# Phase angles by batch: the shared middle tile multiplied and transposed in two 64-row halves

## The chip, the cores and the metric

The kernel runs on one core of one Trainium2 chip. The metric is the device time of one execution in microseconds (us), lower is better. The kernel before takes 2743.87 us (median of 3 runs, 2742.2 to 2744.56). Engines are named as the profile names them: PE is TensorE (its matmuls), PEld are TensorE's weight loads, DVE is VectorE, ACT is ScalarE, POOL is GpSimd, SP is SyncE, which issues most DMAs.

## The reference, cut to what matters

```python
# x: (4, 4224, 192); weight: (8, 7)
def _attn_ref(x, weight):            # causal 7-tap convolution along the sequence, taps softmaxed, one set per head
    ...
def _moe_ref(x, w_theta, w_tok_r, w_tok_i, w_ch):
    theta = x @ w_theta              # (4, 4224, 192): the phase angles
    zr = x * np.cos(theta)
    zi = x * np.sin(theta)
    y = w_tok_r @ zr + w_tok_i @ zi  # two 4224 x 4224 token mixings, for each batch
    u = x + y
    return u + np.maximum(u @ w_ch, 0.0)
def _moe2_ref(x, U, V, w_ch1, w_ch2):
    h = x.transpose(0, 2, 1) @ U @ V # low rank (32) token mixing
    u = x + h.transpose(0, 2, 1)
    return u + np.maximum(u @ w_ch1, 0.0) @ w_ch2   # 192 -> 768 -> 192

out = _moe2_ref(_moe_ref(_attn_ref(x, weight), ...), ...)
```

The change touches only the angles `x @ w_theta` and the token-major copy of `x` that is multiplied with their sine and cosine. Everything is float32.

## The kernel before

**Layout.** The four batches are handled as two pairs. A pair has 2 x 192 = 384 channels, which lie on three tiles of 128 partitions: tile 0 holds channels 0 to 127 of the first batch, tile 1 (the shared one) channels 128 to 191 of the first batch on partitions 0 to 63 and channels 0 to 63 of the second on partitions 64 to 127, tile 2 channels 64 to 191 of the second batch. Tokens run along the free dimension. `Y` keeps the running sum for all four batches and 4224 tokens in SBUF.

**Three stages.** (1) From 0 to about 2130 us 385 steps (`STAGES`) of the token mixing: each step multiplies one operand `z_op` (tokens as the contraction) with one block of weights, as 27 float32r matmuls (lines 1276 to 1278: high x high, high x low, low x high part). Odd and even steps take PSUM banks 0 to 2 and 3 to 5. ACT writes the high part of the weights (line 586), DVE the low part (line 943), DVE adds the finished banks to `Y` (lines 969 to 983). The order of all work on all engines is written out by stage number. (2) The channel mixing `u @ w_ch` and the projection on U (lines 1292 to 1327). (3) The second channel network (lines 1356 to 1375).

**The work around the change.** The operands are prepared in 22 groups of 384 tokens of one pair (`GP`), each in three units of 128 tokens (`KC`), 66 units in all, spread over the steps of stage 1 up to 1886 us. DVE computes the convolution into `attn` (lines 868 and 871); for unit m PE runs `theta(n, r)`, all in plain float32, which PE executes as two records for each matmul, each with a weight load of its own, and as one record for each transpose:

- line 1220: tile 1 (all 128 rows) with `theta_w[:, D:3D]` into all 384 columns of the angle bank; this part of the matrix has the first batch's weights on rows 0 to 63 and columns 0 to 191, the second's on rows 64 to 127 and columns 192 to 383, and zeros elsewhere
- line 1221: tile 0 into columns 0 to 191; line 1224: tile 2 into columns 192 to 383
- line 1226: three transposes of `attn` tiles into the x bank; the last one releases ACT.

Then ACT rounds the angles to turns (`turn`, lines 605 and 608), DVE reduces them (`angles`, lines 907 to 911), ACT computes sines (`sin`, lines 615 to 620) and DVE multiplies them with the x bank (`products`, lines 920 and 922). The results go to DRAM and come back as the operands of later steps. Units 0, 1 and 2 run before the first step, their banks are listed in `theta_bank` and `x_bank`; all later units use bank 6 for the angles and bank 7 for x. A unit waits for the products of the unit before (`pe.wait_ge(product, 2 * m)`). The two float32 convolution tiles that PE computes at the start are line 1234, in `conv_pe`.

One other place has a 64-row matmul: `spread_g` (line 1312), run twice in the whole kernel, multiplies `spread` (64 partitions, 96 columns) with `g_parts` in plain float32. `low_rank` (line 1308) contracts over 96 partitions.

Of the kernel before, what the change touches and what calls it, by code (L numbers as in the profile page):

```python
# [8 lines left out]
ACT = mybir.ActivationFunctionType  # L9
ALU = mybir.AluOpType  # L10
AX = mybir.AxisListType

P = 128
BATCH, SEQ, D = 4, 4224, 192
TAPS, HEADS, RANK, FF = 7, 8, 32, 768
PAIRS = BATCH // 2
TP = 2 * D // P
TILES = PAIRS * TP
TOK_TILES = SEQ // P
GW = 384  # L20
# [10 lines left out]
INV_2PI = float(np.float32(1 / (2 * np.pi)))  # L31
ROUND = 12582912.0
TWO_PI_A = 6.28125
# [70 lines left out]
def splits_done(o):  # L104
    return KC * (o + 1) if o < PIECED else KC * PIECED + o - PIECED + 1
# [54 lines left out]
def conv_done(n):  # L160
    return 2 * TAPS * (n + 1) if n < 2 else 4 * TAPS + CONV * (n - 1)
# [60 lines left out]
def zf_index(m):  # L222
    return m if m < KC else (m % 2 if m < FIRST_UNITS else 0)


def zf_stores(m):
    same = [i for i in range(min(m, FIRST_UNITS - 1) + 1) if zf_index(i) == zf_index(m)]
    return len(same) + max(m - FIRST_UNITS + 1, 0)


def unit_before(m):
    return m - KC + 1 if m == KC - 1 else m - 1
# [31 lines left out]
def build(nc, w_tok, xin, taps_w, w_theta, w_ch, u, v3, w1, w2, ident_in, spread_in, z_out, out):  # L264
    top = ExitStack()
    with top:
        def sb(stack, name, shape, dt=F32):
            return stack.enter_context(nc.sbuf_tensor(name, shape, dt))

        def sem(name):  # L270
            return top.enter_context(nc.semaphore(name))

        psum = top.enter_context(nc.psum_tensor("bank", [P, 8, 512], F32))
# [3 lines left out]
        ident = sb(top, "ident", [P, P])  # L277
# [4 lines left out]
        theta_w = sb(prep, "theta_w", [P, 4 * D])  # L282
# [3 lines left out]
        angle = sb(prep, "angle", [P, GW])  # L286
# [82 lines left out]
        angle_step = sem("angle_step")  # L369
        sin_step = sem("sin_step")  # L370
        product = sem("product")
# [54 lines left out]
        def zf_of(m):  # L426
            return (zf, zf_1, z_raw[:, 1])[zf_index(m)]

        def turns_of(m):
            return turns_1 if m == 1 else turns  # L430

        def angle_of(m):
            return sines_1[:, 0] if m == 1 else angle

        def sines_of(m):
            return sines_1 if m == 1 else sines

        def theta_bank(m):
            return psum[:, {1: 3, 2: 5}.get(m, 6), 0:GW]

        def x_bank(m):
            return psum[:, {1: 4, 2: 2}.get(m, 7), 0:GW]


        @block.sync
# [130 lines left out]
        def _(act):  # L576
# [24 lines left out]
            def turn(m):  # L601
                act.wait_ge(theta_ready, m + 1)
                if m >= 2:
                    act.wait_ge(angle_step, 3 * unit_before(m) + 3)
                nc.scalar.activation(turns_of(m)[:], theta_bank(m), ACT.Copy, scale=INV_2PI,
                                     bias=ROUND).then_inc(turn_step, 1)
                act.wait_ge(turn_step, 2 * m + 1)
                nc.scalar.activation(turns_of(m)[:], turns_of(m)[:], ACT.Copy, bias=-ROUND).then_inc(turn_step, 1)
# [49 lines left out]
            for n, t in enumerate((2, 0)):  # L658
                for k in range(TAPS):
                    nc.scalar.activation(diag[n][:, k], ident[:], ACT.Copy,  # L660
                                         scale=tap[:, t, k:k + 1]).then_inc(diag_ready, 1)
            nc.scalar.activation(sines[:, 0, 0:1], tap[:, 0, 0:1], ACT.Sin).then_inc(table_ready, 1)
            w_hi(0)
            copy_conv(0)
            turn(0)
            turn(1)
            sin(0)
            turn(2)
            piece_hi(0, 0)
            copy_conv(1)  # L670
# [163 lines left out]
        def _(dve):  # L834
            vec = nc.vector
# [64 lines left out]
                        vec.tensor_tensor(h, h, there, ALU.add).then_inc(residual, 1)  # L900

            def angles(m):
                theta, a, t = theta_bank(m), angle_of(m), turns_of(m)
                dve.wait_ge(turn_step, 2 * m + 2)
                if m >= 2:
                    dve.wait_ge(sin_step, 4 * unit_before(m) + 2)
                vec.scalar_tensor_tensor(a[:], t[:], -TWO_PI_A, theta, ALU.mult, ALU.add).then_inc(angle_step, 1)
                dve.wait_ge(angle_step, 3 * m + 1)
                vec.scalar_tensor_tensor(a[:], t[:], -TWO_PI_B, a[:], ALU.mult, ALU.add).then_inc(angle_step, 1)
                dve.wait_ge(angle_step, 3 * m + 2)  # L910
                vec.tensor_scalar(a[:], a[:], PI_BELOW, -PI_BELOW, ALU.min, ALU.max).then_inc(angle_step, 1)  # L911

            def products(m):
                x, to, sc = x_bank(m), zf_of(m), sines_of(m)
                dve.wait_ge(sin_step, 4 * m + 2)
                if KC <= m < FIRST_UNITS:
                    dve.wait_ge(zh_ready, splits_done(1))
                if m >= KC:
                    dve.wait_ge(z_stored[zf_index(m)], 16 * (zf_stores(m) - 1))
                vec.tensor_tensor(to[:, 1], x, sc[:, 0], ALU.mult).then_inc(product, 1)  # L920
                dve.wait_ge(sin_step, 4 * m + 4)
                vec.tensor_tensor(to[:, 0], x, sc[:, 1], ALU.mult).then_inc(product, 1)

            def first_sum(m):
                dve.wait_ge(product, 2 * (m + 1))
# [67 lines left out]
            for k in range(TAPS):  # L993
                conv(0, k)
            w_lo(0)
            angles(0)
            angles(1)
            products(0)
            piece_lo(0, 0)
            angles(2)  # L1000
            products(1)
            piece_lo(0, 1)
            products(2)
            piece_lo(0, 2)
            w_lo(1)
# [104 lines left out]
            for t in range(TU + 1):  # L1110
# [11 lines left out]
                if t < TU:  # L1122
                    g, p = TAIL[t]
# [83 lines left out]
        def _(pe):  # L1207
            mm = nc.tensor.matmul

            def theta(n, r):  # L1210
                m = KC * n + r
                src = attn_1 if n == 1 else attn
                rows = slice(r * P, (r + 1) * P)
                angle_bank, x = theta_bank(m), x_bank(m)
                pe.wait_ge(conv_tap, conv_done(n))
                if n == 1:
                    pe.wait_ge(attn_ready, 2)
                if m >= KC:
                    pe.wait_ge(product, 2 * m)
                mm(angle_bank, src[:, 1, rows], theta_w[:, D:3 * D], start=True, stop=False)  # L1220
                mm(angle_bank[:, 0:D], src[:, 0, rows], theta_w[:, 0:D], start=False, stop=False)
                if n == 0:
                    pe.wait_ge(attn_ready, 1)
                mm(angle_bank[:, D:GW], src[:, 2, rows], theta_w[:, 3 * D:4 * D], start=False, stop=True)
                for t in range(TP):
                    last = nc.tensor.transpose(x[:, t * P:(t + 1) * P], src[:, t, rows], ident[:])
                last.then_inc(theta_ready, 1)

            def conv_pe(n):
# [10 lines left out]
            for r in range(KC):  # L1240
                theta(0, r)
            conv_pe(1)

            for s, (c, q, g) in enumerate(STAGES):
                for n in range(1, GP):
                    for r in range(KC):
                        if theta_stage(n, r) == s:
                            theta(n, r)
# [11 lines left out]
                for k, j in order:  # L1260
# [11 lines left out]
                    rows = slice(j * P, (j + 1) * P)  # L1272
                    to = bank[TP * (s % 2) + j][:, 0:n]
# [4 lines left out]
                    last = mm(to, zl, wh, start=False, stop=(k == KC - 1), skip_group_check=goes_on)  # L1278
# [36 lines left out]
            for t in range(TU):  # L1315
                pe.wait_ge(ul_ready, t + 1)
                for o in range(TP):
# [5 lines left out]
                    for n, a in ins:  # L1323
# [3 lines left out]
                        last = mm(dst, ch_l[:, n], uh, start=False, stop=((n, a) == ins[-1]))  # L1327
# [133 lines left out]
```

## Time and profile before

| | |
|---|---|
| median of 3 runs | 2743.87 us (2742.2 to 2744.56) |
| profiled execution | 2744.39 us |
| its span, first to last instruction | 2742.6 us |
| mean granted TensorE clock | 0.999 of full speed |
| PE busy | 2719.9 us, 99% of the span, 14519 records |
| weight loads busy | 2558.6 us |
| DVE busy | 2138.4 us, 78% |
| ACT busy | 1034.2 us, 38% |

The span is the time from the first to the last instruction on the chip; the profiled execution's own time is 1.8 us more. PE's time includes the pipeline: a matmul's record is longer than the distance to the next record's start, so the durations of records overlap. The chain of work that ended last gives distances between ends instead.

### The profile page before, as it was taken

How to read it: one execution, taken by the hardware profiler on the slowest of the kernel's cores; microseconds unless marked ns; L12 is line 12 of the kernel's file. 1: busy time of each engine (PE TensorE's matmuls, PEld its weight loads, DVE VectorE, ACT ScalarE, POOL GpSimd, SP SyncE). 2: the span in 40 equal slices, each digit the busy share in tenths (PEclk: the TensorE clock that was granted, in tenths of full speed). 3: DMA queues.
4: the chain of work that ended last, by engine and by line, in shares of the span. 5: the costliest groups of instructions: out<-in, count | busy, mean ns of one | idle time of the engine just before them, and what ended most of it. 6: DMA issues, size and time to landing. Idle time of an engine off the chain costs nothing.

```text
span 2742.6 us, 35836 instructions
## 1 busy us (share of the span) xinstructions
PE 2719.9 (99%) x14519; PEld 2558.6 (93%) x14519; DVE 2138.4 (78%) x2473; ACT 1034.2 (38%) x1392; POOL 195.4 (7%) x228
## 2 busy tenths in 40 slices
PE   8999999999999999999999999999999999999999
PEld 7898999999999999999999999999999999999999
DVE  6888977888788788888887997986767876666665
ACT  6543333333333333333333333333332443344343
POOL 0101001001011011010010010100100000000000
PEclk9999999999999999999999999999999999999999
DMA  6878769678677687696686786875962000000000
GB/s 196 203 183 217 174 194 210 155 203 198 176 201 184 178 203 179 182 219 165 191 200 165 204 189 174 199 195 166 224 156 81 35 3 29 31 29 31 29 31 35
DMA packets 102372, 412.62 MB, mean 150 GB/s; under 512 B 10656, under 2 KB 28736, under 8 KB 102080
## 3 DMA queue, kind: packets, MB, share of 16 engines
q0 software_dynamic: 31680, 151.40, 31.3%
q1 hardware_dynamic: 70528, 258.94, 26.9%
q8 instruction: 115, 1.88, 0.3%
q14 instruction: 49, 0.40, 0.0%
HBM read 371.37 MB, written 38.93 MB: 150 GB/s over the span
## 4 chain that ended last, share of the span: by engine, by line
PE 96%; DVE 2%; issue 1%; ACT 0%; DMA 0%; SPq 0%; DVEq 0%; ACTq 0%
PE bank L1276 24%; PE bank L1278 23%; PE bank L1277 23%; PE bank L1371 2%; PE bank L1375 2%; PE bank L1372 2%; PE bank L1374 2%; PE bank L1373 2%; PE bank L1220 2%; PE bank L1356 2%; PE bank L1359 2%; PE bank L1357 2%; PE bank L1360 1%; PE bank L1358 1%; PE bank L1325 1%; PE bank L1327 1%
## 5 line engine op out<-in xcount | busy, mean ns | idle before, releaser
L1276 PE MATMUL bank<-w_h,z_op 128*128 128x448 f32 (+1 forms) x3465 | 1234.7, 356 | 7.6 <-DVE z_op L931 2.7
L1278 PE MATMUL bank<-w_h,z_op 128*128 128x448 f32 (+1 forms) x3465 | 1228.3, 354 | 0.0
L1277 PE MATMUL bank<-w_l,z_op 128*128 128x448 f32 (+1 forms) x3465 | 1228.2, 354 | 0.0
L586 ACT ACTIVATE w_h<-w_raw 128x1344 fp32r<-128x1344 f32 (+1 forms) x385 | 485.7, 1261 | 1064.4 <-PE bank L1278 929.8
L1276 PEld LDWEIGHTS bank<-w_h,z_op 128*128 128x128 f32 x3465 | 651.9, 188 | 50.0 <-DVE z_op L931 3.0
L1278 PEld LDWEIGHTS bank<-w_h,z_op 128*128 128x128 f32 x3465 | 651.8, 188 | 40.9
L1277 PEld LDWEIGHTS bank<-w_l,z_op 128*128 128x128 f32 x3465 | 652.1, 188 | 39.8
L943 DVE TENSOR_TENSOR w_l<-w_raw,w_h 128x1344 fp32r<-128x1344 f32 (+1 forms) x385 | 567.7, 1475 | 63.0 <-ACT w_h L586 62.2
L561 POOL DMA_DIRECT2D w_raw<-in_w_tok x220 | 192.8, 898 | 1866.7 <-DVE w_l L943 1127.0
L1153 DVE SCALAR_TENSOR_TENSOR hid_l<-bank,hid_h 128x384 fp32r<-128x384 f32 x264 | 144.4, 557 | 153.0 <-ACT hid_h L811 149.7
L979 DVE TENSOR_TENSOR Y<-Y,bank 128x1344 f32<-128x1344 f32 (+1 forms) x105 | 154.7, 1473 | 103.0 <-PE bank L1278 102.3
L811 ACT ACTIVATE hid_h<-bank 128x384 fp32r<-128x384 f32 x264 | 129.5, 490 | 235.1 <-PE bank L1360 235.1
L871 DVE SCALAR_TENSOR_TENSOR attn<-x_win,tap,attn 128x384 f32<-128x384 f32 x384 | 213.9, 615 | 0.0
L981 DVE TENSOR_TENSOR Y<-Y,bank 128x1344 f32<-128x1344 f32 (+1 forms) x50 | 73.7, 1474 | 75.5 <-PE bank L1278 75.5
L977 DVE TENSOR_TENSOR Y<-Y,bank 128x1344 f32<-128x1344 f32 (+1 forms) x55 | 81.0, 1472 | 40.8 <-PE bank L1278 40.1
L971 DVE TENSOR_TENSOR Y<-Y,bank 128x1344 f32<-128x1344 f32 (+1 forms) x55 | 81.0, 1472 | 35.9 <-PE bank L1278 35.8
L615 ACT ACTIVATE sines<-angle 128x384 f32<-128x384 f32 x65 | 34.1, 525 | 191.0 <-DVE angle L911 191.0
L937 DVE TENSOR_TENSOR z_op<-z_raw,z_op 128x1152 fp32r<-128x1152 f32 x74 | 100.2, 1354 | 1.4 <-ACT z_op L647 1.4
L975 DVE TENSOR_TENSOR Y<-Y,bank 128x1344 f32<-128x1344 f32 (+1 forms) x55 | 80.9, 1471 | 18.2 <-PE bank L1278 18.1
L1371 PE MATMUL bank<-hid_h,w_h 128*128 128x384 f32 x264 | 91.4, 346 | 3.1 <-DVE hid_l L1153 3.1
L983 DVE TENSOR_TENSOR Y<-Y,bank 128x1344 f32<-128x1344 f32 (+1 forms) x51 | 74.8, 1467 | 20.4 <-PE bank L1278 20.4
L1356 PE MATMUL bank<-full_h,w_h 128*128 128x384 f32 x264 | 89.8, 340 | 0.0
(132 smaller groups left out, 2956.6 us busy)
## 6 DMA issues: line engine op xcount, KB each, us to landing
w_raw<-in_w_tok SPq DMA_DIRECT2D x220, 672.0 KB, 4.5
w_raw<-in_w_tok POOLq DMA_DIRECT2D x220, 672.0 KB, 6.8
z_raw<-z_out SPq DMA_DIRECT2D x85, 576.0 KB, 6.7
z_out<-zf SPq DMA_DIRECT2D x65, 384.0 KB, 6.5
x_win<-in_xin SPq DMA_DIRECT2D x22, 585.0 KB, 5.9
out<-res SPq DMA_DIRECT2D x22, 576.0 KB, 3.0
v_raw<-in_v SPq DMA_DIRECT2D x11, 144.0 KB, 3.2
w_raw<-in_w SPq DMA_DIRECT2D x1, 1536.0 KB, 7.1
```

Of the source, the lines that this page charges most:

```text
L561: nc.gpsimd.dma_start(w_raw[:, slot].rearrange("p k n -> p (k n)"), w_tok[c, g, ADDED[q]], accum_op=ALU.add).then_inc(w_summed[slot], 16)
L586: nc.scalar.activation(w_h[:, s % WRING, :, 0:n], w_raw[:, SLOT[s], :, 0:n], ACT.Copy).then_inc(wh_ready, 1)
L811: nc.scalar.activation(hid_h[:, f % 4], bank[ring_use(f, last) % 3][:, 0:GW], ACT.Relu).then_inc(relu_hi, 1)
L871: vec.scalar_tensor_tensor(to[:, t], x, tap[:, t, k:k + 1], to[:, t], ALU.mult, ALU.add).then_inc(conv_tap, 1)
L943: vec.tensor_tensor(w_l[:, s % WRING, :, 0:n], w_raw[:, SLOT[s], :, 0:n], w_h[:, s % WRING, :, 0:n].bitcast(F32), ALU.subtract).then_inc(w ...
L979: vec.tensor_tensor(c21, c21, sums, ALU.subtract).then_inc(acc_free, 1)
L1153: vec.scalar_tensor_tensor(hid_l[:, f % 4], bank[ring_use(f, last) % 3][:, 0:GW], 0.0, hid_h[:, f % 4].bitcast(F32), ALU.max, ALU.subtract ...
L1276: mm(to, zh, wh, start=(k == 0 and not goes_on), stop=False, skip_group_check=goes_on)
L1277: mm(to, zh, wl, start=False, stop=False, skip_group_check=goes_on)
L1278: last = mm(to, zl, wh, start=False, stop=(k == KC - 1), skip_group_check=goes_on)
L1356: mm(o, w1_h[:, odd, cols], full_h[:, p, odd], start=True, stop=False)
L1371: mm(full, w2_h[:, ff, whole], hh, start=first, stop=False)
```

## The change

The angle bank and the x bank become two banks, one for each batch of the pair: in each, columns 0 to 191 hold the batch's angles and columns 192 to 383 its x. The one 128-row matmul of the shared tile over 384 columns becomes two 64-row matmuls over 192 columns, next to each other in program order: rows 0 to 63 into the first batch's bank, rows 64 to 127 into the second's. The transpose of the shared tile becomes two transposes of 64 rows into the two banks, also next to each other; the transposes of tiles 0 and 2 follow. ACT and DVE read the two banks with one access pattern in two runs of 192 columns. Units 1 and 2 get banks 2 and 3, and 4 and 5; the others keep banks 6 and 7.

```diff
-        def theta_bank(m):
-            return psum[:, {1: 3, 2: 5}.get(m, 6), 0:GW]
-
-        def x_bank(m):
-            return psum[:, {1: 4, 2: 2}.get(m, 7), 0:GW]
+        def unit_banks(m):
+            a = {1: 2, 2: 4}.get(m, 6)
+            return psum[:, a:a + 2]
+
+        def theta_of(m):
+            return unit_banks(m)[:, :, 0:D]
+
+        def x_of(m):
+            return unit_banks(m)[:, :, D:2 * D]
+
+        def by_batch(ap):
+            return ap.rearrange("p (b d) -> p b d", b=2)
...
-                nc.scalar.activation(turns_of(m)[:], theta_bank(m), ACT.Copy, scale=INV_2PI,
+                nc.scalar.activation(by_batch(turns_of(m)[:]), theta_of(m), ACT.Copy, scale=INV_2PI,
                                      bias=ROUND).then_inc(turn_step, 1)
...
-                vec.scalar_tensor_tensor(a[:], t[:], -TWO_PI_A, theta, ALU.mult, ALU.add).then_inc(angle_step, 1)
+                vec.scalar_tensor_tensor(by_batch(a[:]), by_batch(t[:]), -TWO_PI_A, theta, ALU.mult,
+                                         ALU.add).then_inc(angle_step, 1)
...
-                vec.tensor_tensor(to[:, 1], x, sc[:, 0], ALU.mult).then_inc(product, 1)
+                vec.tensor_tensor(by_batch(to[:, 1]), x, by_batch(sc[:, 0]), ALU.mult).then_inc(product, 1)
                 dve.wait_ge(sin_step, 4 * m + 4)
-                vec.tensor_tensor(to[:, 0], x, sc[:, 1], ALU.mult).then_inc(product, 1)
+                vec.tensor_tensor(by_batch(to[:, 0]), x, by_batch(sc[:, 1]), ALU.mult).then_inc(product, 1)
...
-                angle_bank, x = theta_bank(m), x_bank(m)
+                angle, x = theta_of(m), x_of(m)
+                halves = (slice(0, 64), slice(64, P))
...
-                mm(angle_bank, src[:, 1, rows], theta_w[:, D:3 * D], start=True, stop=False)
-                mm(angle_bank[:, 0:D], src[:, 0, rows], theta_w[:, 0:D], start=False, stop=False)
+                mm(angle[:, 0], src[:, 0, rows], theta_w[:, 0:D], start=True, stop=False)
                 if n == 0:
                     pe.wait_ge(attn_ready, 1)
-                mm(angle_bank[:, D:GW], src[:, 2, rows], theta_w[:, 3 * D:4 * D], start=False, stop=True)
-                for t in range(TP):
-                    last = nc.tensor.transpose(x[:, t * P:(t + 1) * P], src[:, t, rows], ident[:])
+                mm(angle[:, 1], src[:, 2, rows], theta_w[:, 3 * D:4 * D], start=True, stop=False)
+                for b, half in enumerate(halves):
+                    mm(angle[:, b], src[half, 1, rows], theta_w[half, (1 + b) * D:(2 + b) * D], start=False, stop=True)
+                for b, half in enumerate(halves):
+                    nc.tensor.transpose(x[:, b, P * (1 - b):P * (1 - b) + 64], src[half, 1, rows], ident[half, half])
+                nc.tensor.transpose(x[:, 0, 0:P], src[:, 0, rows], ident[:])
+                last = nc.tensor.transpose(x[:, 1, 64:D], src[:, 2, rows], ident[:])
                 last.then_inc(theta_ready, 1)
```

## Rows read from the trace of the kernel before

**Rows 1.** The page, busy time by engine and the granted clock in 40 slices.

```profile
PE 2719.9 (99%) x14519; PEld 2558.6 (93%) x14519; DVE 2138.4 (78%) x2473; ACT 1034.2 (38%) x1392; POOL 195.4 (7%) x228
...
PEclk9999999999999999999999999999999999999999
```

**Rows 2.** Stretches: PE, PEld, DVE, ACT, POOL busy (records), PEclk, DMA share, GB/s.

```profile
32.00:600.00 568.00, 563.37 (x2939) 522.87 (x2939) 473.30 (x519) 232.99 (x274) 53.92 (x62) 1.00 0.76 194
600.00:1886.00 1286.00, 1286.00 (x6739) 1199.82 (x6738) 1075.55 (x1085) 460.15 (x528) 121.54 (x139) 1.00 0.75 188
```

**Rows 3.** Chain that ended last around one unit: start, us between ends, what.

```profile
1005.05 0.65 PE bank L1220 x2
1005.70 0.33 PE bank L1221 x2
1006.02 0.33 PE bank L1224 x2
1006.35 0.33 PE bank L1226 x3
1006.67 0.20 PE bank L1276
```

**Rows 4.** The unit's lines, all units: ns of a record min/median/max, first and last start.

```profile
L1220 PE MATMUL bank<-theta_w,attn x132: 483/486/488, 13.5 to 1884.7; 128*128 128x384 f32 x132
...
L1224 PEld LDWEIGHTS bank<-theta_w,attn x132: 189/190/191, 14.3 to 1885.3; 128*128 128x128 f32 x132
...
L1226 PEld LDWEIGHTS bank<-ident,attn x198: 139/141/142, 14.7 to 1885.8; 128*128 128x128 f32 x198
```

**Rows 5.** Chain that ended last around the first 64-row matmul, line 1312.

```profile
2208.43 0.17 PE bank L1302
2208.60 0.81 PE bank L1312 x2
2209.41 0.38 PE bank L1325
2209.79 0.18 PE bank L1326
```

**Rows 6.** The same chain around the second one.

```profile
2257.48 0.81 PE bank L1312 x2
2258.29 0.38 PE bank L1356
2258.67 0.18 PE bank L1357
```

**Rows 7.** Weight loads in order of time around the first: start, us, [idle before].

```profile
2208.53 0.24 PEld L1312 LDWEIGHTS bank<-g_parts,spread 64*96 64x96 f32 x2 [0.30 <-issue]
2209.34 0.19 PEld L1325 LDWEIGHTS bank<-u_h,ch_h 128*128 128x128 f32 x1 [0.57 <-issue]
```

**Rows 8.** PE records around a 96-row matmul (line 1308), in order of time.

```profile
2220.62 0.34 PE L1302 MATMUL bank<-vt_l,u_s 128*64 128x384 f32 x1
2220.79 0.34 PE L1308 MATMUL bank<-v_s,g_s 96*128 96x384 f32 x1
2220.97 0.34 PE L1325 MATMUL bank<-u_h,ch_h 128*128 128x384 f32 x1
```

**Rows 9.** Line 1312's weight loads, all of them.

```profile
L1312 PEld LDWEIGHTS bank<-g_parts,spread x4: 156/158/159, 2208.5 to 2257.5; 64*96 64x96 f32 x4
```

**Rows 10.** Groups by line and shape, DVE and ACT: count, busy us, mean ns, idle before.

```profile
L979 DVE TENSOR_TENSOR Y<-Y,bank 128x1344 f32<-128x1344 f32 x84 | 130.5, 1553 | 66.7 <-PE bank L1278 65.9 <-DVE Y L897 0.2
...
L907 DVE SCALAR_TENSOR_TENSOR angle<-turns,bank 128x384 f32<-128x384 f32 x65 | 35.6, 548 | 2.3 <-ACT turns L608 2.2
...
L605 ACT ACTIVATE turns<-bank 128x384 f32<-128x384 f32 x66 | 32.0, 484 | 16.1 <-PE bank L1226 16.1
```

**Rows 11.** The start in order of time: the units' first matmuls and ACT's copy.

```profile
13.52 0.81 PE L1220 MATMUL bank<-theta_w,attn 128*128 128x384 f32 x2
13.72 0.49 ACT L652 ACTIVATE attn<-bank 128x384 f32<-128x384 f32 x1 [1.07 <-PE bank L1234]
```

**Rows 12.** PE's waits from 80 to 1886 us: total us, times, longest.

```profile
PE bank L1276 <- DVE z_op L937: 2.2, 1, 2.2
PE bank L1276 <- DVE w_l L943: 1.5, 1, 1.5
```

More of the change, by code:

```diff
@@ L902, in angles @@
             def angles(m):
-                theta, a, t = theta_bank(m), angle_of(m), turns_of(m)
+                theta, a, t = theta_of(m), angle_of(m), turns_of(m)
                 dve.wait_ge(turn_step, 2 * m + 2)
@@ L913, in products @@
             def products(m):
-                x, to, sc = x_bank(m), zf_of(m), sines_of(m)
+                x, to, sc = x_of(m), zf_of(m), sines_of(m)
                 dve.wait_ge(sin_step, 4 * m + 2)
```

## The prediction

> **What bounds the kernel now.** I read the page first: PE is busy for 99% of the span at full clock [rows 1]. Then the stretches: from 600 to 1886 us PE has no idle time at all, and from 32 to 600 us it is idle for 568.00 - 563.37 = 4.6 us [rows 2]. DVE is busy for 84% of the second stretch, ACT for 36%. All 66 units of the change lie before 1886 us, and 63 of them behind the start, so almost every unit costs exactly what PE spends on it: the reader should see that a term on PE is multiplied by 66 and nothing hides it, while a term on ACT or DVE is multiplied by nothing unless it is large.
>
> What a unit costs stands in the chain that ended last: 0.65 us for the shared tile (two records over 384 columns), 0.33 and 0.33 for tiles 0 and 2, 0.33 for the three transposes, together 1.64 us, and the token mixing resumes at its normal 0.20 us a matmul without a gap [rows 3]. So 192 columns cost 0.33 / 2 = 0.16 us a record, 384 columns 0.33, and a transpose of 128 columns 0.11. These distances equal streaming time; the records themselves last longer (486 ns against 0.33), because the pipeline overlaps them, and the weight loads (190 ns, 141 for a transpose) are begun behind the matmul before [rows 4]. That last point is what the change touches.
>
> **Part 1: columns streamed.** The shared tile was 2 records x 0.33 = 0.65 us. It becomes 4 records x 0.16 = 0.65 us if they run one after another. Its transpose was one of 128 columns, 0.11 us; it becomes two of 64, 2 x 0.055 = 0.11. Tiles 0 and 2 and their transposes stay as they are. So without any overlap between halves, streaming saves nothing. The saving must come from matmuls that run side by side in different halves of the array's rows. No row of the trace shows two such matmuls, so I bound it. From one side: no overlap, 0. From the other: each half hides the other whole, which saves 0.33 us on the matmuls and 0.05 on the transposes, 0.38 together. Between them I go by program order. A plain float32 matmul is two records, each with its own load [rows 4]; so the order on PE is first half record 1, first half record 2, second half record 1, second half record 2, then first transpose, second transpose. If starts keep that order, records 1 and 2 of the same half cannot run together, and only neighbours of different halves can: record 2 of the first half with record 1 of the second (saves 0.16), and record 2 of the second half with the first transpose (saves 0.05). I take 0.16 + 0.05 = 0.21 us for a unit, close to the middle of the two ends.
>
> The Trainium skill, "TensorEngine Tiling (Array Packing)", section Theoretical Speedup, gives up to 2x for a contraction of at most 64 rows. Taken at its full value that is the 0.38 us end, and the sum below would come out at about zero; no row here shows it.
>
> **Part 2: going into 64 rows and back.** The trace of before has a matmul that does just this, twice: line 1312, 64 rows, plain float32, 384 columns, between 128-row matmuls. Its two records take 0.81 us of the chain where line 1220's two with as many columns take 0.65 [rows 3, 5, 6]: +0.16 for going in. The 128-row matmul behind it takes 0.38 where its neighbours take 0.17 to 0.18: +0.21 for coming back [rows 5, 6]. The weight loads say why: both the 64-row load and the first 128-row load behind it begin only after an idle time (0.30 and 0.57 us), not behind the running matmul [rows 7]. So at each change the array runs empty and the load is exposed. It is not the semaphore wait before it: line 1308, with 96 rows and waits of its own, follows its neighbours at the usual 0.17 and 0.18 us [rows 8].
>
> The Trainium skill, same page, section Key Properties, says that changing the tiling mode drains TensorE; it gives no figure, and the trace agrees with the 0.37 us above.
>
> Carried to a unit, going in loads 128 columns and not 96, 190 against 158 ns [rows 4, 9]: 0.16 + 0.03 = 0.19. Coming back, the first load is that of a transpose, 141 against 190 ns [rows 4]: 0.21 - 0.05 = 0.16. A unit goes in once and comes back once (tiles 0 and 2, then both half matmuls and both half transposes, then the full transposes), so +0.35 us. The bounds: 0.37 as measured, and below, if a stream of plain float32 on both sides drains faster than the mixed one of the rows, perhaps only the two exposed loads of 0.11 and 0.05 (a record less its 0.08 us of latency, by the distance of load starts), 0.16.
>
> **Part 3: ACT and DVE.** They read two runs of 192 columns in two banks instead of one of 384. An addition over three banks takes 1553 ns for 1344 elements and line 907 takes 548 for 384 from one bank [rows 10]: the difference is 1005 ns for 960 elements, 1.05 ns each, so crossing banks adds nothing that shows. I cost it at 0. If it did cost some 60 ns on each of four instructions, DVE has 210 us of idle time between 600 and 1886 us [rows 2], which hides it; with that cover gone it would be 66 x 0.2 = 13 us.
>
> **Part 4: waits.** Unit 0 needs tile 2, which ACT copies from 13.72 to 14.21 us. Before, 0.65 + 0.33 us of other matmuls lay ahead of its use; now only tile 0's 0.33, so PE waits from about 13.85 to 14.25: +0.4 us, once [rows 11]. Units 1 and 2, then the second convolution, are queued behind it, and the start is a chain through them, so it counts in full. Later units keep their wait on the products of the unit before; the new banks of units 1 and 2 are those that the first two steps wait for anyway.
>
> Against this, PE's few waits for DVE in the first 600 us (the two longest are 2.2 and 1.5 us [rows 12]) shrink a little if PE itself is later there. I take -0.6 us of 4.6.
>
> **The sum.** A unit: +0.35 - 0.21 = +0.14 us. 66 x 0.14 = 9.2 us, +0.4 at the start, -0.6: +9.0 us. The profiled execution took 2744.4 us, 0.5 above the median of the runs, so I forecast 2753 us, 0.3% slower.
>
> **Rivals.**
> A. No overlap: the halves run one after another. 66 x 0.35 = 23.1 us, 2767 us. For it: nothing in the trace shows float32 matmuls side by side. A dearer form, each switch of half exposing a load (0.11 + 2 x 0.05 more), gives 66 x 0.56 = 37 us, 2781.
> B. Full overlap: 0.35 - 0.38 = -0.03 us a unit, -2 us, 2742, no change. Against it: two records of one half lie next to each other.
> C. The other side: the drain is cheap. If going in and out costs only the loads, 0.16 us, and halves overlap by 0.21 to 0.38, a unit saves 0.05 to 0.22 us: 3 to 14 us, at its likeliest 2734. It decides as soon as the round trip is cheaper than the overlap. Against it: the 0.37 us stands twice, at two places with different neighbours, to 0.01 us.
> D. The halves are not run as 64-row work at all, but like the 96-row matmul without a drain and without overlap: no change, 2744. Against it: line 1312 has 64 rows and drains.
>
> **How the numbers follow.** Runs spread over 0.09%; about 0.2%, 5.5 us, is what can be told from no change. Forecast 0.48 (of this, a tenth within 0.2%, should the overlap be larger), A 0.24 and its dearer form 0.04, B 0.08, C 0.12 (a quarter of it within 0.2%), D 0.04. Slower: 0.43 + 0.28 = 0.71; same 0.05 + 0.08 + 0.04 + 0.03 = 0.20; faster 0.09. The range goes from B, 2741, to A with its uncertainty, 2769; outside are most of C and A's dearer form. The forecast's own range is 2749 to 2758.
>
> **What would show it.** Per unit, in the chain: tiles 0 and 2 at 0.33 each; the 64-row records together near 0.19 + 0.65 - 0.16 us; the last two transposes near 0.22 + 0.16. Weight loads with idle time before the first half matmul and before the first full transpose, 2 a unit. Two 64-row records that start closer than 0.16 us would show the overlap; all at 0.16 would be A. DVE's and ACT's means should stay at 548 ns and 484 ns [rows 10]. I am wrong if those loads are begun early (C, D), or if the records of both halves start in pairs (B).

## The result and the profile after

The changed kernel takes 2748.13 us (median of 19 runs, 2746.64 to 2750.7) against 2743.87 us before (19 runs, 2742.2 to 2747.0): ratio 1.0016, 95% interval 1.0010 to 1.0023. It is slower by 4.3 us, 0.16%. That lies in the wide range (2741 to 2769), but just below the forecast's own range of 2749 to 2758. It is on the forecast's side, but half of its +9 us, and by the prediction's own bound of 0.2% it counts as no change. The profiled execution took 2747.45 us with a span of 2745.7 us, 3.1 us more than before.

The page first, busy time by engine and the clock; then the stretches that answer to [rows 1] and [rows 2].

```profile
PE 2723.9 (99%) x14717; PEld 2547.6 (93%) x14717; DVE 2138.7 (78%) x2473; ACT 1034.9 (38%) x1392; POOL 195.1 (7%) x228
...
PEclk9999999999999999999999999999999999999999
```

```profile
32.00:600.00 568.00, 564.01 (x3014) 520.64 (x3013) 473.63 (x518) 233.16 (x274) 54.90 (x63) 1.00 0.77 194
600.00:1886.00 1286.00, 1286.00 (x6829) 1188.71 (x6828) 1073.57 (x1083) 459.09 (x526) 120.36 (x137) 1.00 0.75 187
```

PE still has no idle time from 600 to 1886 us. The 198 more records are the 3 more of each of 66 units. DVE's and ACT's totals moved by 0.3 and 0.7 us.

Now one unit in the chain that ended last, as in [rows 3]: start, us between ends, what.

```profile
1004.42 0.20 PE bank L1291
1004.62 0.33 PE bank L1230 x2
1004.95 0.33 PE bank L1233 x2
1005.27 0.53 PE bank L1235 x4
1005.80 0.06 PE bank L1237 x2
1005.86 0.26 PE bank L1238
1006.12 0.11 PE bank L1239
1006.22 0.20 PE bank L1289
```

From 1004.62 to 1006.22 it is 1.60 us, where the unit before took 1.62, from 1005.05 to 1006.67 [rows 3]. So the unit became *cheaper*, not dearer by 0.14. Next come the weight loads around it in order of time, then all records of the half matmuls (ns min/median/max), then the first two of them in this unit:

```profile
1005.20 0.30 PEld L1235 LDWEIGHTS bank<-theta_w,attn 64*128 64x128 f32 x4 [0.23 <-issue]
1005.47 0.14 PEld L1237 LDWEIGHTS bank<-ident,attn 64*128 64x128 f32 x2
1005.78 0.14 PEld L1238 LDWEIGHTS bank<-ident,attn 128*128 128x128 f32 x1 [0.17 <-issue]
```

```profile
L1235 PE MATMUL bank<-theta_w,attn x264: 322/375/427, 14.0 to 1888.5; 64*128 64x192 f32 x132
```

```profile
1005.20 0.43 PE L1235 MATMUL bank<-theta_w,attn 64*128 64x192 f32 x2
```

Call it a change of mode when PE goes from 128-row to 64-row work or back. Both changes show as forecast: a load behind idle time before the first half matmul (0.23 us) and before the first full transpose (0.17 us). The four half records take 0.53 us of the chain. What was not forecast is the last line: two records together fill 0.43 us, and one alone lasts up to 427 ns, so they run almost exactly on top of each other. The trace's single start times say it for every unit: the four records start in two pairs, 7 ns apart within a pair. The second pair starts 0.27 us behind the first, which carries the exposed load of the way in; the half transposes start 0.16 us behind the second pair, which is streaming alone, and 7 ns apart too. The overlap is full.

If each unit is cheaper by 0.02 us, 66 of them should save 1.4 us. Where do 3.1 us more come from? I set the starts of the 10395 matmuls of the token mixing side by side. Up to 640 us the changed kernel is ahead, by 1.85 us at the 111th step. From there it falls back by 0.4 us in each group of four steps, twice in every 35, and at 1920 us it is 3.06 us behind. These losses do not lie at the units but in ordinary steps of mixing. Here is line 1291 (before: 1278) in such a stretch, and in the same one before:

```profile
L1291 PE MATMUL bank<-w_h,z_op x30: 368/368/368, 838.6 to 856.6; 128*128 128x448 f32 x30
```

```profile
L1278 PE MATMUL bank<-w_h,z_op x30: 362/366/370, 839.8 to 857.4; 128*128 128x448 f32 x30
```

Every third matmul is of this line, so 30 starts span 29 x 3 matmuls: 18.0 us / 87 = 206.9 ns after, 17.6 us / 87 = 202.3 ns before. The durations are a signature: at the usual pace they wander between 362 and 370 ns, and the starts repeat a pattern near 207, 202, 203, 202, 199 ns, 202.7 on average; at the slow pace all are 368, and the starts lie at 206, 207, 207 ns. I call a step slow if its matmuls of 448 columns lie over 205 ns apart on average, counted from the third matmul on, so that the handover from a unit does not weigh in, and leaving out the one or two steps with a wait inside. Of 308 steps of this width, 2 are slow before and 63 after. One costs 27 x 4.0 ns = 0.107 us.

Neither the clock nor the load of the DMA engines tells the two apart. Here is the same stretch after and before: PE, PEld, DVE, ACT, POOL busy (records), PEclk, DMA share, GB/s.

```profile
838.50:857.00 18.50, 18.50 (x91) 16.80 (x90) 15.57 (x20) 6.35 (x9) 2.80 (x3) 1.00 0.85 197
```

```profile
839.50:858.00 18.50, 18.50 (x93) 17.16 (x92) 15.85 (x20) 6.45 (x9) 2.80 (x3) 1.00 0.85 200
```

The granted clock is 1.00 in both, and the DMA engines are busy for 0.85 of both stretches.

The account of the spans is then: units 66 x -0.022 = -1.45 us, slow steps 61 x 0.107 = +6.5 us, and -2.0 us left over to reach the measured +3.1. Of this remainder 0.8 us is there by the second step, and another 0.7 us is one wait for DVE at 171 us that is gone; the rest I did not trace.

### The profile page after: what moved, and what is told of

Same layout as the page of the kernel before. It is cut to its first block, busy times and chain, and to the rows that moved or that the text cites. A ratio compares the mean times of both kernels' runs of the same rounds, so it can differ in the third digit from the quotient of the medians.

```text
span 2745.7 us, 36232 instructions
## 1 busy us (share of the span) xinstructions
PE 2723.9 (99%) x14717; PEld 2547.6 (93%) x14717; DVE 2138.7 (78%) x2473; ACT 1034.9 (38%) x1392; POOL 195.1 (7%) x228
## 4 chain that ended last, share of the span: by engine, by line
PE 97%; DVE 2%; issue 0%; ACT 0%; DMA 0%; SPq 0%; DVEq 0%; ACTq 0%
PE bank L1289 24%; PE bank L1291 24%; PE bank L1290 24%; PE bank L1384 2%; PE bank L1388 2%; PE bank L1387 2%; PE bank L1385 2%; PE bank L1386 2%; PE bank L1369 2%; PE bank L1372 2%; PE bank L1373 1%; PE bank L1371 1%; PE bank L1370 1%; PE bank L1235 1%; PE bank L1338 1%; PE bank L1340 1%
```

## The experiments

For each I give the time, the cost of a unit and the number of slow steps, the last two worked out from the start times in the trace. The cost of a unit is the distance from the last mixing matmul ahead of it to the second one behind it, less two matmuls at their usual pace, as a median of the units behind 600 us. Each ratio is to runs of the kernel before taken alongside (medians 2743.5 to 2744.0).

| kernel | time, us | ratio to before, 95% | span, us | unit, us | slow steps |
|---|---|---|---|---|---|
| before | 2743.87 | | 2742.6 | 1.622 | 2 |
| changed | 2748.13 | 1.0016 (1.0010 to 1.0023) | 2745.7 | 1.600 | 63 |
| one_half | 2767.51 | 1.0086 (1.0070 to 1.0101) | 2765.3 | 1.982 | 2 |
| tr_halves | 2760.87 | 1.0061 (1.0046 to 1.0076) | 2759.3 | 1.881 | 9 |
| apart | 2812.02 | 1.0247 (1.0232 to 1.0263) | 2808.4 | 2.659 | 3 |
| after_dup | 2751.39 | 1.0030 (1.0018 to 1.0041) | 2748.7 | 1.710 | 6 |
| before_dup | 2750.80 | 1.0029 (1.0018 to 1.0039) | 2749.0 | 1.735 | 15 |
| halves_first | 2745.21 | 1.0005 (0.9996 to 1.0014) | 2742.8 | 1.650 | 0 |
| halves_last | 2749.74 | 1.0021 (1.0012 to 1.0030) | 2748.1 | 1.648 | 42 |
| full_around | 2743.25 | 0.9997 (0.9988 to 1.0006) | 2740.7 | 1.601 | 6 |
| second_first | 2748.19 | 1.0015 (1.0006 to 1.0025) | 2745.7 | 1.599 | 64 |
| full_swapped | 2748.39 | 1.0017 (1.0008 to 1.0026) | 2745.7 | 1.599 | 61 |
| before_432 | 2751.25 | 1.0026 (1.0015 to 1.0036) | 2750.0 | 1.621 | see text |

### Is the gain of a unit the overlap?

**one_half.**

```diff
-                for b, half in enumerate(halves):
+                for b, half in enumerate((halves[0], halves[0])):
```

(in both loops, matmuls and transposes)

> The changed kernel with both half matmuls and both half transposes taken from rows 0 to 63 (the second batch's share of the middle tile is computed from the wrong rows). The same number of 64-row records, but none can run beside another. Theory (the gain is overlap of two halves; going into 64 rows and back costs 0.35 us): the unit is 1.60 us in the changed kernel and here 1.60 + 0.33 + 0.05 = 1.98 us, 66 units, +25 us against the changed kernel, about 2773 us. Rival (the 64-row records are short for another reason, for instance fewer rows stream faster): the unit stays at 1.60 us and the time at 2748 us.

Measured: 2767.51 us, unit 1.98 us, as the theory said. In its chain:

```profile
1018.06 0.84 PE bank L1235 x4
1018.91 0.12 PE bank L1237 x2
```

0.84 against 0.53 us, 0.12 against 0.06: with both halves on the same rows the four records no longer fit on each other. That is 0.31 + 0.06 us of overlap in the chain and 0.38 by the start times, where 0.33 + 0.05 is all that full overlap can give. The rival is out. On the same rows no two of the half matmuls' records start closer than 0.16 us, so the pairs 7 ns apart in the changed kernel must hold one record of each half.

**tr_halves.** Only the transposes have 64 rows.

```diff
-                for b, half in enumerate(halves):
-                    mm(angle[:, b], src[half, 1, rows], theta_w[half, (1 + b) * D:(2 + b) * D], start=False, stop=True)
+                for b in range(2):
+                    mm(angle[:, b], src[:, 1, rows], theta_w[:, (1 + b) * D:(2 + b) * D], start=False, stop=True)
```

> The changed kernel with the two half matmuls made of 128 rows again (two matmuls of 192 columns, the zeros of the matrix included); only the two transposes have 64 rows. Theory (round trip 0.35 us, matmul overlap worth 0.33, transposes 0.05): the unit is 1.60 + 0.33 = 1.93 us, 0.30 over the kernel before, +20 us, 2764 us, plus whatever steps of the token mixing run at 206.7 ns a matmul. Rival (the round trip is much cheaper than 0.35 us, and the overlap worth less): the unit is near 1.75 us and the time near 2752 us.

Measured: 2760.87 us, unit 1.88 us, 0.26 over before, between the theory's 1.93 and the rival's 1.75 and nearer to the theory.

```profile
916.99 0.65 PE bank L1235 x4
917.64 0.21 PE bank L1237 x2
917.84 0.26 PE bank L1238
918.11 0.11 PE bank L1239
```

The chain says where the missing 0.05 us went. Two half transposes take 0.21, of which 0.055 is streaming, so the way in costs 0.15 here, with a transpose's load exposed, against 0.20 in the changed kernel (0.53 - 0.33) with a matmul's. The way back is 0.26 - 0.11 = 0.15 in both. So this round trip costs 0.30. The price depends on which loads it exposes, as the prediction had it, and I had left that out of this expectation.

**apart.** Three trips, halves not next to each other.

```diff
+                mm(angle[:, 0], src[halves[0], 1, rows], theta_w[halves[0], D:2 * D], start=True, stop=False)
-                mm(angle[:, 0], src[:, 0, rows], theta_w[:, 0:D], start=True, stop=False)
+                mm(angle[:, 0], src[:, 0, rows], theta_w[:, 0:D], start=False, stop=True)
...
+                mm(angle[:, 1], src[halves[1], 1, rows], theta_w[halves[1], 2 * D:3 * D], start=True, stop=False)
-                mm(angle[:, 1], src[:, 2, rows], theta_w[:, 3 * D:4 * D], start=True, stop=False)
-                for b, half in enumerate(halves):
-                    mm(angle[:, b], src[half, 1, rows], theta_w[half, (1 + b) * D:(2 + b) * D], start=False, stop=True)
+                mm(angle[:, 1], src[:, 2, rows], theta_w[:, 3 * D:4 * D], start=False, stop=True)
```

> The changed kernel with the halves' matmuls set apart: first half, tile 0, second half, tile 2, then the half transposes and the full ones. Three trips into 64 rows and back instead of one, and no two half matmuls next to each other. Theory: 1.60 + 2 x 0.35 (trips) + 0.33 (lost overlap) = 2.63 us a unit, +1.0 us over before, 66 us, about 2810 us. Rival (the halves overlap although a 128-row matmul stands between them, or a trip costs less in plain float32): below 2790 us.

Measured: 2812.02 us, unit 2.66 us, where the theory said 2.63. A unit in its chain:

```profile
1041.11 0.52 PE bank L1230 x2
1041.63 0.52 PE bank L1231 x2
1042.15 0.52 PE bank L1234 x2
1042.67 0.52 PE bank L1235 x2
1043.19 0.20 PE bank L1237 x2
1043.40 0.26 PE bank L1238
```

Lines 1230 and 1234 are the half matmuls, 1231 and 1235 the full ones. Each takes 0.52 us where streaming takes 0.33, so a matmul's load costs 0.20 us on the way in and 0.20 on the way out: 0.39 us (before rounding) for each of the first two trips. The third, between transposes, costs 0.15 + 0.15 = 0.30. The mean is near 0.35 us, but no single trip costs that. A 128-row matmul between two halves takes their overlap away.

### What sets the slow pace?

**after_dup.** The changed kernel's last transpose twice.

```diff
-                last = nc.tensor.transpose(x[:, 1, 64:D], src[:, 2, rows], ident[:])
+                for _ in range(2):
+                    last = nc.tensor.transpose(x[:, 1, 64:D], src[:, 2, rows], ident[:])
```

> The changed kernel with its last transpose issued twice, which shifts only the moment at which a unit ends: +0.11 us a unit, 7.2 us. In the changed kernel 63 steps of the token mixing run at 206.7 ns a matmul instead of 202.7, which costs 0.107 us a step, 6.7 us; before there were 2 such steps. Theory (the pace is set by the phase, of a few ns, in which the unit hands over to the mixing): the number of slow steps changes much, to near 0 or to above 100; near 0 the time is 2748 + 7.2 - 6.7 = 2748 to 2749 us. Rival (64-row work or the new banks slow what follows): still 63 slow steps, 2755 us.

Measured: 2751.39 us, 6 slow steps in place of 63. 66 more records of 0.11 us, 7.2 us of work, lengthen the span by only 3.1 us; 57 x 0.107 = 6.1 us went with the slow steps, and some 2 us came in places that I did not trace. 64-row work and the new banks are all still there, so they do not cause the slow pace by themselves.

**before_dup.** The same in the kernel before.

```diff
-                for t in range(TP):
+                for t in (0, 1, 2, 2):
```

> The kernel before, with its last transpose issued twice: the same shift of a unit's end without any 64-row work and with the old banks. +0.11 us a unit, 7.2 us. Theory (the slow pace comes from the phase of the handover alone): the number of slow steps may leave its 2 of before; at n slow steps the time is 2744 + 7.2 + 0.107 (n - 2) us, so 2751 us at 2 and 2758 us at 63. Rival (the slow pace needs 64-row work or the new banks): 2 slow steps again, 2751 us. Only a large number tells them apart for certain.

Measured: 2750.80 us, 15 slow steps. Line 1278 in one of these stretches:

```profile
L1278 PE MATMUL bank<-w_h,z_op x9: 365/368/369, 129.0 to 134.0; 128*128 128x448 f32 x9
```

The same signature without any 64-row work and with the old banks. The number rose from 2 to 15, all ahead of 500 us, not to the large one that I had asked for. The kernel before says the same by itself: its 2 slow steps begin behind a wait for DVE, with no unit there.

```profile
97.75 0.44 PE L1276 MATMUL bank<-w_h,z_op 128*128 128x448 f32 x1 [1.52 <-DVE w_l L943]
```

So 64-row work is not needed for the slow pace. By after_dup it is not enough for it either, nor by one_half and apart, with 2 and 3 slow steps. What these runs share is that they move the moment at which the mixing resumes.

**second_first and full_swapped.** The halves in the other order; the last two transposes in the other order.

```diff
-                for b, half in enumerate(halves):
+                for b, half in ((1, halves[1]), (0, halves[0])):
```

```diff
-                nc.tensor.transpose(x[:, 0, 0:P], src[:, 0, rows], ident[:])
-                last = nc.tensor.transpose(x[:, 1, 64:D], src[:, 2, rows], ident[:])
+                nc.tensor.transpose(x[:, 1, 64:D], src[:, 2, rows], ident[:])
+                last = nc.tensor.transpose(x[:, 0, 0:P], src[:, 0, rows], ident[:])
```

> The changed kernel with the two halves in the other order (rows 64 to 127 first), in the matmuls and the transposes. Nothing else. Theory: the halves overlap in the same way, the unit is 1.60 us; the handover may fall a few ns away from that of the changed kernel, and the slow steps are then not 63. If the phase is the same to the ns, everything is the same, 2748 us. Rival (the order of the halves matters for their overlap): the unit changes by 0.1 us or more.

> The changed kernel with its last two transposes in the other order (tile 2, then tile 0). Same shapes, same places for loads; only banks and addresses differ. Theory (phase in time alone): the same 1.60 us and the same 63 slow steps, 2748 us. Rival (the bank or address of the last record matters for the pace of what follows): another number of slow steps, down to 2742 us.

Measured: 2748.19 and 2748.39 us, 64 and 61 slow steps, units of 1.599 us, spans equal to the changed kernel's to 0.1 us. The rows, banks or addresses of the records change, the timing does not, and the number of slow steps hardly does.

### Can the unit be arranged better?

**halves_first and halves_last.** The 64-row work at the head and at the end of a unit.

```diff
+                for b, half in enumerate(halves):
+                    nc.tensor.transpose(x[:, b, P * (1 - b):P * (1 - b) + 64], src[half, 1, rows], ident[half, half])
+                for b, half in enumerate(halves):
+                    mm(angle[:, b], src[half, 1, rows], theta_w[half, (1 + b) * D:(2 + b) * D], start=True, stop=False)
-                mm(angle[:, 0], src[:, 0, rows], theta_w[:, 0:D], start=True, stop=False)
+                mm(angle[:, 0], src[:, 0, rows], theta_w[:, 0:D], start=False, stop=True)
...
-                mm(angle[:, 1], src[:, 2, rows], theta_w[:, 3 * D:4 * D], start=True, stop=False)
-                for b, half in enumerate(halves):
-                    mm(angle[:, b], src[half, 1, rows], theta_w[half, (1 + b) * D:(2 + b) * D], start=False, stop=True)
-                for b, half in enumerate(halves):
-                    nc.tensor.transpose(x[:, b, P * (1 - b):P * (1 - b) + 64], src[half, 1, rows], ident[half, half])
+                mm(angle[:, 1], src[:, 2, rows], theta_w[:, 3 * D:4 * D], start=False, stop=True)
```

```diff
+                nc.tensor.transpose(x[:, 0, 0:P], src[:, 0, rows], ident[:])
+                if n == 0:
+                    pe.wait_ge(attn_ready, 1)
+                nc.tensor.transpose(x[:, 1, 64:D], src[:, 2, rows], ident[:])
                 mm(angle[:, 0], src[:, 0, rows], theta_w[:, 0:D], start=True, stop=False)
-                if n == 0:
-                    pe.wait_ge(attn_ready, 1)
                 mm(angle[:, 1], src[:, 2, rows], theta_w[:, 3 * D:4 * D], start=True, stop=False)
...
                 for b, half in enumerate(halves):
-                    nc.tensor.transpose(x[:, b, P * (1 - b):P * (1 - b) + 64], src[half, 1, rows], ident[half, half])
-                nc.tensor.transpose(x[:, 0, 0:P], src[:, 0, rows], ident[:])
-                last = nc.tensor.transpose(x[:, 1, 64:D], src[:, 2, rows], ident[:])
+                    last = nc.tensor.transpose(x[:, b, P * (1 - b):P * (1 - b) + 64], src[half, 1, rows], ident[half, half])
```

> The changed kernel with the 64-row work at the head of a unit: half transposes, half matmuls, then tiles 0 and 2 and their transposes, so that a unit ends as it did before, with two 128-row transposes behind 128-row matmuls, and tile 2 is needed later in unit 0. Same records, one trip into 64 rows. Theory: the unit stays at 1.60 us (the load exposed on the way in is that of a transpose, on the way out that of a matmul: the sum is the same); the start gains up to 0.5 us; slow steps few, as before (2), because the handover is that of before: 2744 - 1.4 - 0.5 = 2742 us. Rival (any 64-row work in the unit leaves the slow pace behind it): some 63 slow steps, 2748 us.

> The changed kernel with the 64-row work at the end of a unit: the two full transposes, the two full matmuls, the half matmuls, the half transposes, and the token mixing straight behind them. The load that is exposed on the way out is then the mixing's first, which is 0.08 us late behind a transpose anyway. Theory: the unit is 1.60 - 0.03 = 1.57 us, 66 units, 2 us less than 1.60 us gives: 2740 us with few slow steps, 2747 us with 63. Rival (the way out costs 0.21 us and the 0.08 us as well): 1.65 us, 3 us more.

Measured: 2745.21 us with 0 slow steps and a unit of 1.650 us; 2749.74 us with 42 and 1.648 us. Of the first, the few slow steps were forecast and the unit was not, and its time can't be told from before (ratio 1.0005, 0.9996 to 1.0014). Its chain shows the place:

```profile
907.04 0.21 PE bank L1231 x2
907.25 0.38 PE bank L1233 x4
907.63 0.52 PE bank L1234 x2
```

The half matmuls take 0.38 us where streaming takes 0.33. I put the 0.05 us down to a matmul's load that does not fit behind a transpose of 64 columns; no other run shows it. In halves_last the first matmul of the mixing takes 0.40 us in place of 0.20:

```profile
911.76 0.06 PE bank L1239 x2
911.81 0.40 PE bank L1289
```

0.20 us for the way out, dearer than the 0.15 of the changed kernel, and nothing is saved elsewhere: the rival held. In the changed kernel the 0.08 us by which the first mixing matmul's record is longer behind a transpose is not a cost at all; the chain gives it 0.20 us, like any other.

**full_around.** One full transpose moved to the head.

```diff
+                nc.tensor.transpose(x[:, 0, 0:P], src[:, 0, rows], ident[:])
                 mm(angle[:, 0], src[:, 0, rows], theta_w[:, 0:D], start=True, stop=False)
...
-                nc.tensor.transpose(x[:, 0, 0:P], src[:, 0, rows], ident[:])
                 last = nc.tensor.transpose(x[:, 1, 64:D], src[:, 2, rows], ident[:])
```

> The changed kernel with one of its two full transposes (tile 0) moved from behind the half transposes to the head of the unit: the same records, one trip into 64 rows, but only one 128-row transpose between it and the token mixing, so the handover falls in another phase. Theory (unit 1.60 us, and the phase of the handover decides how many steps run at 206.7 ns): the number of slow steps is not 63; with none the time is 2744 - 1.4 - 0.4 + 0 = 2741 to 2742 us, and this beats both kernels by a hair. Rival (with one transpose only, the mixing's first weight load is exposed further): the unit is 1.65 us and more, 3 us more.

Measured: 2743.25 us, ratio 0.9997 (0.9988 to 1.0006), unit 1.601 us, 6 slow steps; the rival (a unit of 1.65 us) is out. It has the changed kernel's work to the record and is 4.9 us faster in the median, 5.0 us in the span. Line 1291 where the changed kernel is slow:

```profile
L1291 PE MATMUL bank<-w_h,z_op x29: 361/366/369, 838.5 to 855.6; 128*128 128x448 f32 x29
```

Against before its time is not measurably different. Its profiled span is 1.9 us shorter; the account above gives -1.45 for the units and +0.4 for 4 more slow steps, and the rest is not traced. That is about what the change is worth when few steps are slow.

**before_432.** Is the pace a matter of the width 448?

```diff
-TW = 448
+TW = 432
```

> The kernel before with the token mixing's blocks 432 columns wide and the last one 384 instead of 448 and 320: the same columns and the same number of matmuls. In the trace a matmul of 320 columns takes 146.5 ns = 320 / 2.4 + 13.2, one of 448 takes 202.7 = 448 / 2.4 + 16.0 at its usual pace and 206.7 = 448 / 2.4 + 20.0 at the slow one. Theory (the overhead belongs to the phase between weight loads and matmuls, and 448 columns fit it badly): 432 / 2.4 + 13.2 = 193.2 ns and 173.2 ns; a chunk of 35 steps then costs 27 x 7 x (4 x 193.2 + 173.2) against 27 x 7 x (4 x 202.7 + 146.5), 2.1 us less, 11 chunks, 23 us: 2721 us. Rival (the overhead grows with the columns): 432 columns at 195.5 ns, 384 at 174.6 ns: no change.

Measured: 2751.25 us, slower. Away from the handovers, matmuls of 432 columns lie 196.8 ns apart (432 / 2.4 + 16.8), those of 384 174.9 (384 / 2.4 + 14.9), and in the kernel before those of 320 146.7 (320 / 2.4 + 13.3). The theory is wrong and the rival right that the overhead grows with the columns, at least from 320 to 432 (at 448 it is 16.0), and even it was too kind: 4 x 196.8 + 174.9 = 962.1 ns against 4 x 202.7 + 146.7 = 957.5, which for 11 chunks of 27 x 7 is 9.6 us more. The span grew by 7.4; I did not trace the difference. Of these two splits the one of the kernel before is the better.

## Why the prediction held, and where it did not

**What bounds the kernel:** right. PE has no idle time from 600 to 1886 us, and every one of these kernels follows its unit. With u the unit in us and s the slow steps, 2742.6 + 66 (u - 1.622) + 0.107 (s - 2) is worked out for the eleven kernels with this block width besides before. It lies 0.1 to 2.7 us above each measured span, over a stretch of 68 us. (The prediction adds a unit up to 1.64 us from rounded rows; its own chain, 1005.05 to 1006.67, gives 1.62.)

**Part 2, going into 64 rows and back:** right, mechanism and size. Forecast 0.19 + 0.16; in the chain 0.20 + 0.15, and 0.36 together by the start times (-0.022 + 0.380). The price came from two instances of another 64-row matmul [rows 5, 6], corrected for the loads exposed. The correction is borne out too: apart and tr_halves show 0.39 us for a trip with a matmul's load at both ends and 0.30 with a transpose's.

**Part 1, columns streamed:** this step failed. I took 0.21 us of overlap, because "record 2 of the first half with record 1 of the second" seemed the only pair that could meet. The records start in pairs, 7 ns apart, which is the prediction's own sign for rival B, and one_half puts the overlap at 0.38 us, so the end "each half hides the other whole" is the true one. What was wrong was the premise "if starts keep that order": a record of each half starts before either half's second record does. Whether the records reach PE in another order or PE starts them in another order, no run tells. So the unit's term was +0.14 forecast and -0.02 measured, which is rival B almost to the 0.01 us. The Trainium skill, "TensorE: Matmul & The Clock Gate", section Part 3: Packing small matmuls, has matmuls on different row groups run at once, starting some 4 ns apart. The trace agrees that they run at once, with starts 7 ns apart here, and shows it for plain float32 with its two records as well.

**The term that was missing:** the pace of the mixing behind a unit. No step of the prediction had it. It is 61 steps x 0.107 us = +6.5 us and alone makes the change slower. Rival B with this term is what happened: -1.5 + 6.5 - 2. So that the time came out slower, as forecast, and near the forecast's own range was luck: a unit term too high by 10.7 us (66 x 0.162) and a missing one of 6.5 us partly cancelled. Its trace was there before the prediction: the kernel before has 2 slow steps, at 98 to 109 us, but in its sum they weigh 0.2 us.

**Part 3, ACT and DVE:** right. Line 915 (before: 907) and line 613 (before: 605):

```profile
L915 DVE SCALAR_TENSOR_TENSOR angle<-turns,bank 128x384 f32<-128x384 f32 x65 | 35.7, 548 | 2.0 <-ACT turns L616 1.9
...
L613 ACT ACTIVATE turns<-bank 128x384 f32<-128x384 f32 x66 | 32.0, 485 | 15.8 <-PE bank L1239 15.8
```

548 and 485 ns, against 548 and 484 in [rows 10]. (The price for the other case was summed wrongly: four times 60 ns are 0.24 us a unit and 16 us, not 13. Nothing turned on it.)

**Part 4, waits:** half right. The wait of unit 0 is there:

```profile
13.45 0.30 PEld L1233 LDWEIGHTS bank<-theta_w,attn 128*128 128x128 f32 x2 [0.35 <-ACT attn L660]
```

It costs 0.35 us, yet the first mixing matmul starts at 22.26 us instead of 22.62. The work ahead of unit 0 is the same, but its end moved from 13.7 to 12.9 us, and over all these kernels the first mixing matmul starts between 21.9 and 25.5 us, with before_dup, which has more work ahead of it, at 22.15. So 0.4 us at the start is below what one profile can tell. The shrinking of PE's waits was in the sum as -0.6 us, and PE's idle time from 32 to 600 us did fall from 4.6 to 4.0 us. But the reason given, that PE would be later there, does not hold: PE was 0.8 us ahead when the wait at 171 us went away. Why it went is not shown.

**What stays open:** why PE keeps two paces for 448 columns. In the changed kernel 16 of the 17 runs of slow steps begin right behind a unit and one behind 0.27 us of idle time; 15 end at the next block of 320 columns and two at a later unit. Two units of the changed kernel, at 813.1 and 836.6 us, agree in all starts to 4 ns up to the second matmul of the mixing; behind it the first goes on at 196 and 199 ns and the second at 207 and 206. Which of these ns decide, and between which of PE's parts, no run tells. after_dup, before_dup, full_around and the two swaps leave the timing of the handover as the one cause that fits them all: what changes it changes the number of slow steps, and what leaves it alone does not. No run moved the timing and nothing else, and the mechanism is not shown.

## What to carry to other kernels

Two float32 matmuls of 64 rows next to each other, on different rows and banks, overlap fully here; but each trip into 64 rows and back cost 0.30 to 0.39 us on a PE that is never idle, by the loads that it exposed. It pays only if the overlap saves more than that: here 0.38 us were saved for 0.36 spent. Price a mode change from any place in the trace where the mode already changes, and keep the order so that the loads it exposes are small ones. When a change to a saturated engine is worth a few tenths of a per cent, compare the pace of the instructions it did not touch before believing the sum over those it did: here they moved the time by more than four times as much, the other way.

## What was not expected of the hardware

- 128x448 float32r matmuls, back to back and with no wait, have two stable paces, 202.7 and 206.7 ns (durations 362 to 370 ns, or 368 throughout), at the same granted clock of 1.00. Two handovers that agree to 4 ns are followed by different ones. In this kernel family 0 to 64 of 308 steps of this width ran at the slow one, worth up to 6.9 us of 2743.
- The overhead on top of the columns at 2.4 GHz is not the same for all widths: 13.3 ns at 320, 14.9 at 384, 16.8 at 432, 16.0 or 20.0 at 448.
- Full overlap holds for the two-record float32 form, in pairs 7 ns apart, and for half transposes.
- A trip from 128 rows into 64 and back has no single price: 0.30 us between transposes, 0.36 in by a matmul and out by a transpose, 0.39 between matmuls.
